# A fused attention and two-layer MLP kernel: places of weight units, layout of the kept attention output, first loads, and one square root, all moved

## What is computed

```
state = gamma[h] * state + k[t] v[t]^T ;  y[t] = q[t] @ state / sqrt(D)      # decayed linear attention
x = y as (3072 tokens, 512)
x = relu(x @ w_in)**2 @ w_out                       # first layer,  d_ff 2048
xn = x / sqrt(mean(x*x) + 1e-6) * rms_g
out = (silu(xn @ w_gate) * (xn @ w_val)) @ w_out2   # second layer, d_ff 1536
```

## Time and profile before

| | |
|---|---|
| median of 3 runs | 1126.97 us (1125.06 to 1131.64) |
| the profiled execution | 1123.85 us, its span 1122.1 us |
| PE busy | 1092.1 us, 97% |
| DVE, ACT, POOL busy | 871.8, 571.1, 352.7 us |
| DMA | 195.91 MB, 175 GB/s over the span |
| mean granted TensorE clock | 0.998 |

### The profile page before, as it was taken

How to read it: one execution, slowest core, us unless ns; L and a number is a source line. 1 busy time by engine, 2 the same in 40 slices (tenths; PEclk the granted TensorE clock), 3 DMA queues, 4 the chain that set the end, 5 groups by cost and what they waited for, 6 DMA issues and landing times.

```text
span 1122.1 us, 15891 instructions
## 1 busy us (share of the span) xinstructions
PE 1092.1 (97%) x6190; PEld 934.8 (83%) x6190; DVE 871.8 (78%) x933; ACT 571.1 (51%) x768; POOL 352.7 (31%) x260
## 2 busy tenths in 40 slices
PE   7998999999999999999998999999999999999998
PEld 6887877888788888788887788998888998888898
DVE  4787988978969878879888776977667877766683
ACT  1333656466545556554566455455545455454452
POOL 2786553002441004440014444003444102444000
PEclk9999999999999999999999999999999999999999
DMA  9999556763545563445633324462212564120355
GB/s 353 375 384 364 202 194 214 270 219 106 186 168 207 189 205 119 182 188 191 218 135 134 130 76 183 155 207 76 75 38 103 217 203 135 38 76 1 113 189 169
DMA packets 60234, 195.91 MB, mean 175 GB/s; under 512 B 5760, under 2 KB 20224, under 8 KB 54784
## 3 DMA queue, kind: packets, MB, share of 16 engines
q1 hardware_dynamic: 51712, 190.70, 48.0%
q10 hardware_dynamic: 8448, 4.20, 1.3%
HBM read 152.41 MB, written 42.47 MB: 174 GB/s over the span
## 4 chain that ended last, share of the span: by engine, by line
PE 82%; DMA 7%; DVE 6%; issue 3%; ACT 3%; SPq 0%; POOL 0%; ACTq 0%; DVEq 0%; POOLq 0%
PE Y L686 9%; PE Y L688 9%; PE Y L687 9%; PE Z L688 6%; PE Z L687 6%; PE Z L686 6%; PE X L686 6%; PE X L688 6%; PE X L687 6%; DMA x_scratch<-y_sb 4%; PE Y L772 2%; PE Y L768 2%; PE Y L770 2%; PE Z L768 2%; PE X L770 2%
## 5 line engine op out<-in xcount | busy, mean ns | idle before, releaser
L565 POOL TENSOR_TENSOR w_ops<-raw_w,w_ops 128x512 fp32r<-128x512 f32 x90 | 126.2, 1402 | 503.8 <-ACT w_ops L818 503.4
L872 ACT CAST ops<-hid 128x1024 fp32r<-128x1024 f32 x147 | 154.1, 1048 | 166.2 <-PE Y L688 32.8
L1153 DVE TENSOR_TENSOR ops<-hid,ops 128x1024 fp32r<-128x1024 f32 x147 | 179.9, 1224 | 53.7 <-ACT ops L872 53.3
L565 POOL TENSOR_TENSOR w_ops<-sums_w,w_ops 128x512 fp32r<-128x512 f32 x120 | 166.4, 1388 | 147.1 <-ACT w_ops L818 146.8
L686 PE MATMUL Y<-ops,w_ops 128*128 128x512 f32 x360 | 142.1, 395 | 10.4 <-ACT u L900 6.0
L687 PE MATMUL Y<-ops,w_ops 128*128 128x512 f32 x360 | 140.4, 390 | 0.0
L688 PE MATMUL Y<-ops,w_ops 128*128 128x512 f32 x360 | 140.3, 390 | 0.0
L818 ACT CAST w_ops<-sums_w 128x512 fp32r<-128x512 f32 x120 | 74.3, 620 | 48.6 <-PE Y L688 27.6
L909 ACT ACTIVATE gt<-gt 128x512 f32<-128x512 f32 x72 | 45.1, 633 | 97.6 <-DVE gt L1384 37.7
L686 PE MATMUL X<-ops,w_ops 128*128 128x512 f32 x240 | 94.7, 395 | 0.0
L688 PE MATMUL X<-ops,w_ops 128*128 128x512 f32 x240 | 93.5, 389 | 0.0
(11 more groups left out here) (164 smaller groups left out, 2658.7 us busy)
## 6 DMA issues: line engine op xcount, KB each, us to landing
ops<-item_scratch SPq DMA_DIRECT2D x147, 512.0 KB, 3.6
raw_w<-w_f SPq DMA_DIRECT2D x30, 1024.0 KB, 4.9
chunk<-qkv SPq DMA_DIRECT2D x48, 512.0 KB, 8.9
item_scratch<-hid SPq DMA_DIRECT2D x28, 512.0 KB, 2.8
item_scratch<-ops SPq DMA_DIRECT2D x14, 512.0 KB, 8.8
y_scratch<-hid SPq DMA_DIRECT2D x12, 512.0 KB, 5.3
raw<-y_scratch SPq DMA_DIRECT2D x3, 2048.0 KB, 9.3
raw<-w_b SPq DMA_DIRECT2D x5, 1024.0 KB, 5.9
```

The source lines that it names most:

```text
L565: nc.gpsimd.tensor_tensor(w_ops[:, k, 1], front_w_source(m, k), f32(w_ops[:, k, 0]), ALU.subtract).then_inc(w_lo, 1)
L872: nc.scalar.copy(hop_at(n)[:, 0], hid[:, 2 * g:2 * g + 2, OPERAND[k], :]).then_inc(hop_hi, 1)
L1153: nc.vector.tensor_tensor(hop[:, 1], hid[:, 2 * g:2 * g + 2, OPERAND[k], :], f32(hop[:, 0]), ALU.subtract).then_inc(hop_lo, 1)
```

## The change

There are five edits.

1. `ITEMS` is reordered from (0, 6, 1, 4, 3, 2, 5) to (0, 1, 6, 4, 2, 3, 5), and the sums of a quad move from units 0, 1, 5, 9 to 0, 1, 4, 8. The waits and the order of items in `item_scratch` follow. In `EARLY`, the two first sums of quad 1 come ahead of the last two units of quad 0.
2. `units_at`: quads 4 and 5 get 6 units a run in place of 8 (slots 1 to 4 hold 1, 2, 2, 1). Quad 6 gets 3 a run over m = 13 to 16. Quads 2 and 3 keep 8 a run.
3. `x_scratch` becomes 16 blocks of one chunk each. A store writes 2 KB contiguous per partition. A front load becomes 16 DMAs (8 chunks by 2 halves), each of two pieces of 512 bytes per partition, all on SP and at the same place of SP's program.
4. k and v of chunk 0 and `decay_k` are issued by ACT at the head of its program. On SP the mask comes second.
5. For the last tile, the Sqrt moves to group 4 of the first back run of layer two, and `inverse` to group 13 of it.

```diff
-ITEMS = (0, 6, 1, 4, 3, 2, 5)
+ITEMS = (0, 1, 6, 4, 2, 3, 5)
 def units_at(m, slot):
-    first, count = ((0, 0), (0, 1), (1, 3), (4, 3), (7, 1), (8, 0), (8, 0))[slot]
     if m < R1:
+        first, count = ((0, 0), (0, 1), (1, 3), (4, 3), (7, 1), (8, 0), (8, 0))[slot]
         quads, x = (2, 3), 8 * (m - 1) + first
     elif m < M1 and m % R1 in (1, 2):
-        quads, x = (R1 + m // R1 - 1,), 8 * (m % R1 - 1) + first
-    elif m in (M1 + 1, M1 + 2):
-        quads, x = (QUADS - 1,), 8 * (m - M1 - 1) + first
+        first, count = ((0, 0), (0, 1), (1, 2), (3, 2), (5, 1), (6, 0), (6, 0))[slot]
+        quads, x = (R1 + m // R1 - 1,), 6 * (m % R1 - 1) + first
+    elif M1 < m < M1 + R2 - 1:
+        first, count = ((0, 0), (0, 1), (1, 1), (2, 1), (3, 0), (3, 0), (3, 0))[slot]
+        quads, x = (QUADS - 1,), 3 * (m - M1 - 1) + first
-    x_dram = nc.dram_tensor("x_scratch", (TILES - 1, P, 2, 2, 2, N), F32, kind="Internal").ap()
+    x_dram = nc.dram_tensor("x_scratch", (16, P, 2, 2, P), F32, kind="Internal").ap()
-        EARLY = [(0, u) for u in range(10)] + [(1, 0), (1, 1), (0, 10)] + [(1, u) for u in range(2, 11)]
+        EARLY = [(0, u) for u in range(9)] + [(1, 0), (1, 1), (0, 9), (0, 10)] + [(1, u) for u in range(2, 11)]
             load_chunk(0, 0, "qk")
-            sp.dma_start(decay_k_sb[:], decay_k).then_inc(decay_k_loaded, 16)
+            sp.dma_start(mask_sb[:], decay_mask).then_inc(mask_loaded, 16)
             load_chunk(0, 1, "qk")
-            sp.dma_start(mask_sb[:], decay_mask).then_inc(mask_loaded, 16)
-            load_chunk(0, 0, "kv")
...
-                    src = x_dram[t - 1].rearrange("p h s k n -> p (h s k n)")
+                    for i, (b, c) in enumerate(stored_chunks()):
+                        tile, half, at = x_place(b, c)
+                        if tile == t:
+                            for h in range(2):
+                                sp.dma_start(raw[:, h, half, :, at:at + P], x_dram[i, :, h]).then_inc(x_loaded, 16)
+                    return
...
-                act.dma_start(x_dram[tile - 1, :, :, half, :, at:at + P],
-                              y_sb[:, i % 3, :].rearrange("p (h k t) -> p h k t", h=2, k=2))\
+                act.dma_start(x_dram[i].rearrange("p h k t -> p (h k t)"), y_sb[:, i % 3, :])\
                     .then_inc(x_stored[i % 3], 16)
...
+                    if bk.second and t == 0 and n == 4:
+                        root(TILES)
...
+            act.dma_start(chunk[:, 0, K:, :], qkv[0, 0, :, K:, :]).then_inc(kv_loaded[0], 16)
+            act.dma_start(decay_k_sb[:], decay_k).then_inc(decay_k_loaded, 16)
             for n in range(NCH):
                 copy_out(n)
...
-                if fresh and t == 0:
-                    inverse(TILES - 1)
...
+                    if bk.second and t == 0 and n == 13:
+                        inverse(TILES - 1)
```

More of the change, by code:

```diff
@@ L354, in unit_item @@
         def unit_item(unit):
-            return (None, None, 0, 1, 2, None, 3, 4, 5, None, 6)[unit]
+            return (None, None, 0, 1, None, 2, 3, 4, None, 5, 6)[unit]
         def x_place(b, c):
@@ L586, in quad_unit @@
                 A11, A12, A21, A22 = (quad_raw(quad, a) for a in range(4))
-                if unit in (0, 1, 5, 9):
+                if unit in (0, 1, 4, 8):
                     if unit == 0:
@@ L593, in quad_unit @@
                         op = nc.gpsimd.tensor_tensor(quad_sums(quad, 1), A11, A21, ALU.subtract)
-                    elif unit == 5:
+                    elif unit == 4:
                         pool.wait_ge(quad_sum, 4 * quad + 1)
-                        pool.wait_ge(quad_lo, 7 * quad + 3)
+                        pool.wait_ge(quad_lo, 7 * quad + 2)
                         op = nc.gpsimd.tensor_tensor(quad_sums(quad, 0), quad_sums(quad, 0), A11, ALU.subtract)
@@ L599, in quad_unit @@
                         pool.wait_ge(quad_sum, 4 * quad + 3)
-                        pool.wait_ge(quad_lo, 7 * quad + 6)
+                        pool.wait_ge(quad_lo, 7 * quad + 5)
                         op = nc.gpsimd.tensor_tensor(quad_sums(quad, 0), A12, quad_sums(quad, 0), ALU.subtract)
@@ L824, in high_front @@
                     if k == 0:
-                        act.wait_ge(x_loaded, 16 * front)
+                        act.wait_ge(x_loaded, 256 * min(front, 2) + 16 * max(front - 2, 0))
                     if k == 2:
@@ L1002, in front_run, with root @@
                 quads(6)
[L1003 to L1006, removed]
+                if fresh and 0 < front < TILES:
+                    root(front)
+            def root(front):
+                act.wait_ge(ms_saved, front)
+                nc.scalar.activation(rinv_t[:, front - 1, :], ms_t[:], ACT.Sqrt, bias=eps[:, 0:1], scale=1.0 / DM)\
+                    .then_inc(rms_ready, 1)
             def back_run(bk):
@@ L1222, in quad_unit @@
                         op = nc.vector.tensor_tensor(quad_sums(quad, 1), A11, A21, ALU.subtract)
-                    elif unit == 5:
+                    elif unit == 4:
                         dve.wait_ge(quad_sum, 4 * quad + 1)
-                        dve.wait_ge(quad_lo, 7 * quad + 3)
+                        dve.wait_ge(quad_lo, 7 * quad + 2)
                         op = nc.vector.tensor_tensor(quad_sums(quad, 0), quad_sums(quad, 0), A11, ALU.subtract)
@@ L1228, in quad_unit @@
                         dve.wait_ge(quad_sum, 4 * quad + 3)
-                        dve.wait_ge(quad_lo, 7 * quad + 6)
+                        dve.wait_ge(quad_lo, 7 * quad + 5)
                         op = nc.vector.tensor_tensor(quad_sums(quad, 0), A12, quad_sums(quad, 0), ALU.subtract)
```

## The result

| | before | after |
|---|---|---|
| median | 1126.89 us (1125.06 to 1131.64, 4 runs) | 1115.86 us (1115.13 to 1117.18, 4 runs) |
| profiled execution, span | 1123.85, 1122.1 us | 1117.18, 1115.4 us |

The ratio is 0.9897, 95% interval 0.9865 to 0.9929: about 1% faster, 11 us by the medians. The forecast was 1117. The two profiled executions lie only 6.7 us apart: that of before, 1123.85 us, is faster than every timed run of its kernel, that of after the slowest of its own. The sections that follow divide the 6.7 us.

What follows compares the result with a forecast made beforehand. PE bounds the kernel, busy 1092.1 of 1122.1 us, leaving 30.0 us to win. Terms 3.0 + 0.3 + 0.3 + 2.1 + 5.3 + 0 - 1.4 = 9.6 us take the median from 1126.97 to about 1117; range 1111 to 1125.

Steps and rivals of the forecast that it cites:

- Stores, +3.0: Attention: faster stores of outputs end the waits of copies into `y_sb`, winning 3.0 us of PE's 3.52; bounds 0 to 3.5.
- the half us held back for them: Attention: 3.0 taken where all gone wins 3.5, since DVE is nearly as late and already releases PE late.
- First loads, +0.3: Start of attention: k and v of chunk 0 come earlier, but scores 1 precede the state matmuls; +0.3 us, bounds -1.5 to +1.9.
- Runs m = 1 to 3, +0.3: Early layer runs: same eight units a run, only reordered, under gaps of 0.82, 1.06 and 0.98; +0.3 us, bounds -0.7 to +1.1.
- 0.82 stays: Gap at 145.11: the cast of the fifth item still waits for the first item's store, so 0.82 us remains.
- the ring: At 180.52: quad 3's last cast waits in a ring of three for a store, one more store just ahead; -0.5 us.
- Runs m = 4 to 11, +2.1: Runs m = 5, 6, 9, 10: fewer units remove gaps of 1.02 and 1.06 from DVE adding p5 late; bounds +1.0 to +2.1.
- m = 12 to 14, +5.3: Moving the root and loosening units removes gaps of 1.33, 1.74 and 2.21 us; +5.3, bounds +3.5 to +5.3.
- The front load, -1.4: First back run: 16 issues delay item 8, so PE stands 0.8 to 2.0 us before group 8; -1.4 taken.
- the prediction's own signs of being wrong: Gap above 4 us before group 8, copies waiting as before, PE idle above 24 us, or first state matmul after 12 us.
- Rival B: First back run: the front load costs 4 to 6 us, issues of 0.7 us giving a 4.4 us stall; 1120.4 us, chance 0.13.
- The second front: Second back run: the front's 8 us of issues and 3.2 us of landing just fit in some 11 us; counted as hidden.

Runs made afterwards that it cites:

- the kernel with 8 DMAs: The changed kernel with the first front loaded by 8 DMAs of 256 KB in place of 16 of 128 KB, source pieces still 512 bytes; 1111.94 us.
- item 8 alone: The changed kernel with one wait added on SP: item 9 of the first back run is issued only when item 8 has landed; 1114.49 us.

## Why the prediction was right, step by step

**Stores, +3.0.** Right. The waits on stores went, three waits on DVE are there (0.63, 0.76 and 0.58 us) where there had been two, as the half us held back for them said. Undoing the edit costs 2.6 us in attention, and 0.5 in run m = 0. The landing fell from 11.6 to 6.7 us. From the rule of the Trainium skill (DMA: Bandwidth & Descriptors, "Queues, rings and completion order") the prediction had estimated less than half. The direction agrees, the size doesn't, and the waits went all the same.

**First loads, +0.3.** Right in its mechanism: the first state product starts at 11.32 against 11.40, since PE now waits 1.54 us for q and k of chunk 1. PE's first start moved from 4.95 to 5.69, which was allowed for. The gain of 0.3 itself can't be told from the scatter of the start, up to 1.2 us. The cure was in that step's own argument: "q and k of chunk 1 are now behind the mask".

**Runs m = 1 to 3, +0.3.** The sum was near (+0.7), a part wrong: "0.82 stays". The first item's store is issued 4.5 us sooner (132.80 against 137.30), and 3.4 of that is the shift of the whole stage; the cast of the fifth item then no longer waits. At 176.41 the gap grew from 0.98 to 1.71, as said for the ring.

**Runs m = 4 to 11, +2.1, and m = 12 to 14, +5.3.** All gaps named went. The sizes were low, 9.5 us in place of 7.4. The term was read off the list of gaps, and a gap there is short by the matmul's overlap: before 303.58 the last matmul had started at 302.17, so PE's starts are 1.41 us apart where 0.23 is usual, a loss of 1.18, listed as 1.02; with the first matmul behind it slower as well, the seeds moved by 1.45.

**The front load, -1.4.** The mechanism and place were right, the size wrong: -6.9. Its terms one by one. Issues: 8.05 us (forecast 7.7), right. Landing of item 8: 6.0 us where 3.2 to 4.4 was said; the step looked at what is ahead of the item in the queue and not at the two items that its own delay would release with it. The gap came to 4.10 us where 1.4 was said, and above 4 us at this place was one of the prediction's own signs of being wrong. And this standstill then had a price of its own, which wasn't in the sum: the windows of the changed kernel show it.

```profile
206.50:211.00 4.50, 0.40 (x3) 0.10 (x1) 3.50 (x4) 1.96 (x2) 0.00 (x0) 0.84 0.89 313
211.00:213.00 2.00, 2.00 (x5) 1.61 (x6) 0.00 (x0) 0.00 (x0) 0.00 (x0) 0.50 0.84 340
213.00:215.00 2.00, 2.00 (x6) 1.51 (x6) 0.00 (x0) 0.00 (x0) 0.00 (x0) 0.50 0.12 47
215.00:217.00 2.00, 2.00 (x8) 1.59 (x7) 0.00 (x0) 0.58 (x1) 0.00 (x0) 0.65 0.00 0
```

From 210.93 to about 216.2 the granted clock is 0.50, the 1.2 GHz level, and 12 matmuls start 0.43 us apart in place of 0.23: 2.6 us more. From start to start PE stood 4.25 us longer than usual, and the two together are the 6.9 us. In the kernel with 8 DMAs PE stood still for 1.55 us and the clock stayed at 1.00. Rival B had the size of the stall (4.4 us) but not its reason: it took issues of 0.7 us, and they took 0.50. The second front, ahead of all items of its back run, is hidden as said: that stage takes 67.85 us in both kernels. The Trainium skill's rule to coalesce small transfers (DMA: Bandwidth & Descriptors, "Rules for kernel authors") was borne out in part: 16 DMAs in place of one cost 6.9 us where they stood in one block, and nothing where they were spread.

**The whole.** By its terms the forecast of 9.6 us is a sum of misses that cancel: the front took 5.5 us more, and the other stages gave 2.1 (layers), 0.4 (m = 1 to 3) and 0.1 more, which makes the 6.7 of the two profiled executions. Against the medians, 11.0 us, the forecast was nearer (1117 against 1115.86), and that is luck: the front cost 5.5 us more than was said, the other stages won 2.6 more, and the part of the medians' distance that the two traces don't hold made up the rest.

## What to carry to other kernels

When one step of a queue grows, count what becomes ready behind it in the meantime: those transfers go out in a burst, and the one that is needed first lands later than it would by itself (6.0 us against 4.6 here). Put a gap of a few microseconds on TensorE into the sum with the slower matmuls behind it. And when an edit bundles a gain and a loss (here a layout that helps the store and splits the load), undo it alone even if the whole is faster; the loss of 6.9 us was more than twice the gain, and moving the pieces between the item loads kept both.

## What the runs showed of the hardware

- Short standstills and the clock: when PE started again after 4.10 us, the granted clock was 0.50 for 5.3 us. After 2.67 us (item 8 alone) it was 0.55 over 209.25 to 213.00; after 1.55 us (8 DMAs) it was 1.00. The length of one standstill doesn't decide it: after the 2.21 us of the kernel before at 636.67 the clock stayed at 1.00, and after 1.97 us at 85.08 in the kernel whose front has 1 KB pieces it was 0.50. The second line is that one.

```profile
209.25:213.00 3.75, 3.75 (x10) 2.99 (x11) 0.81 (x1) 0.00 (x0) 0.00 (x0) 0.55 0.75 283
...
85.50:88.90 3.40, 3.40 (x25) 2.85 (x25) 2.02 (x3) 1.14 (x2) 2.52 (x3) 0.50 1.05 407
```

- Loads of 512 KB issued 0.5 us apart on one queue land in order, 1.2 to 1.3 us apart (items 8 to 10 of the changed kernel), but the first of them is late: 2.5 us behind the last piece of the front, against 1.3 us with nothing issued after it. The first four items of the back run before, issued about 0.5 us apart, took 4.9, 5.9, 6.6 and 7.2 us where a single one takes 3.2.
- A table load on ACT takes 1.28 us. The Trainium skill (ScalarE: Activation LUTs, "What ACT_TABLE_LOAD costs") has about 1283 ns for it, and the trace agrees; it adds a drain of about 1380 ns, of which the trace shows nothing: the Sqrt starts at 602.74, 1.30 us after the load at 601.44.
- The kernel before varies more than the changed one: 1124.4 to 1131.6 us over its 27 timed runs, against 1115.1 to 1117.2 over four. Its own trace, 1123.85 us, lies below them all. What its slower runs wait for was not seen, as none of them was profiled; this is the greater part of the 4.3 us that the traces don't explain. A candidate is in the two traces with the old stores, where a wait for a copy was followed by a granted clock of 0.50 (88.8 to 92.1 and 85.5 to 88.9 us); the trace of the kernel before has such waits without it.
